# Second network's last tile: four pairs of first-layer products ahead of the projections, which accumulate in another PSUM bank

## The reference, cut to what matters

```python
attn_out = _attn_ref(q, kv, w_sr)      # pooled keys, softmax(q k^T) v: 12288 tokens x 128
h = x @ moe_w_in                       # 12288 x 2048
x = (h * (1.0 / (1.0 + np.exp(-1.702 * h)))) @ moe_w_out     # first network, back to 128
h = x @ moe2_w_in                      # second network
relu6 = np.clip(h + 3.0, 0.0, 6.0)
out = (h * relu6 / 6.0) @ moe2_w_out   # 12288 x 128, float32
```

## Time and profile before

| what | before |
|---|---|
| median of 3 runs | 1310.77 us (1310.31 to 1311.88) |
| the profiled execution, own time | 1312.06 us |
| its span, first to last instruction | 1310.3 us |
| TensorE busy | 1279.5 us, 98% |
| VectorE busy | 1037.8 us, 79% |
| ScalarE busy | 1031.9 us, 79% |
| mean granted TensorE clock | 0.997 of full |

### The profile page before, as it was taken

The page is one execution under the profiler, slowest core; times in us unless marked ns, Lnnn a source line. Parts: engine busy times, 40 slices in busy tenths (PEclk is TensorE's granted clock), DMA queues, the critical chain, the costliest instruction groups (busy, mean ns, idle before and its releaser), DMA issues.

```text
span 1310.3 us, 18296 instructions
## 1 busy us (share of the span) xinstructions
PE 1279.5 (98%) x5748; PEld 1063.1 (81%) x5748; DVE 1037.8 (79%) x1072; ACT 1031.9 (79%) x1211; POOL 36.5 (3%) x43
## 2 busy tenths in 40 slices
PE   6799999999999999999999999999999999999997
PEld 6578888888888888888888888888888888888785
DVE  4777788888878888788888887887788888887666
ACT  2678788788888888788888878888888788788665
POOL 1900000000000000000000000000000000000000
PEclk9999999999999999999999999999999999999999
DMA  9232203213023032131230321311302203102001
GB/s 283 78 72 53 65 9 72 48 24 72 21 51 71 2 72 48 24 72 28 44 72 1 72 52 20 72 36 36 72 9 63 61 11 72 43 21 65 9 1 17
DMA packets 186884, 65.94 MB, mean 50 GB/s; under 512 B 108656, under 2 KB 179440, under 8 KB 186608
## 3 DMA queue, kind: packets, MB, share of 16 engines
q1 hardware_dynamic: 185808, 65.56, 22.2%
q10 hardware_dynamic: 1056, 0.13, 0.1%
HBM read 23.13 MB, written 6.34 MB: 22 GB/s over the span
## 4 chain that ended last, share of the span: by engine, by line
PE 95%; DVE 2%; ACT 1%; DMA 1%; issue 0%; SPq 0%; ACTq 0%
PE pair L796 16%; PE pair L798 16%; PE pair L797 16%; PE bank_av L796 9%; PE bank_av L798 9%; PE bank_av L797 9%; PE bank_out L796 7%; PE bank_out L798 6%; PE bank_out L797 6%; PE pair L810 1%; DMA kv_sb<-in_kv_dram 1%; DVE neg_max L606 0%; ACT work L449 0%; DVE work L665 0%; DVE mid_lo L672 0%
## 5 line engine op out<-in xcount | busy, mean ns | idle before, releaser
L672 DVE TENSOR_TENSOR mid_lo<-work,mid_hi 128x1024 fp32r<-128x1024 f32 (+1 forms) x193 | 235.0, 1218 | 135.2 <-ACT mid_hi L462 135.0
L796 PE MATMUL pair<-x_hi,w_hi 128*128 128x512 f32 x768 | 303.0, 394 | 4.5 <-DVE x_lo L648 3.2
L797 PE MATMUL pair<-x_lo,w_hi 128*128 128x512 f32 x768 | 300.2, 391 | 0.0
L798 PE MATMUL pair<-x_hi,w_lo 128*128 128x512 f32 x768 | 299.9, 390 | 0.0
L434 ACT ACTIVATE work<-pair 128x1024 f32<-128x1024 f32 x192 | 197.1, 1027 | 126.3 <-PE pair L798 123.6
L656 DVE TENSOR_TENSOR mid_lo<-work,mid_hi 128x1024 fp32r<-128x1024 f32 x192 | 236.0, 1229 | 32.3 <-ACT mid_hi L441 32.3
L665 DVE SCALAR_TENSOR_TENSOR work<-work,pair 128x1024 f32<-128x1024 f32 (+1 forms) x193 | 232.5, 1205 | 10.0 <-ACT work L449 9.9
L449 ACT ACTIVATE work<-pair,half 128x1024 f32<-128x1024 f32 (+1 forms) x193 | 212.2, 1100 | 12.4 <-PE pair L798 12.4
L441 ACT ACTIVATE mid_hi<-work 128x1024 fp32r<-128x1024 f32 x192 | 202.6, 1055 | 5.6 <-PE bank_av L798 3.4
L462 ACT ACTIVATE mid_hi<-work 128x1024 fp32r<-128x1024 f32 (+1 forms) x193 | 201.4, 1044 | 0.6 <-DVE work L665 0.6
L796 PEld LDWEIGHTS pair<-x_hi,w_hi 128*128 128x128 f32 x768 | 144.8, 188 | 43.0 <-ACT work L434 7.0
(11 more groups left out here) (87 smaller groups left out, 1507.0 us busy)
## 6 DMA issues: line engine op xcount, KB each, us to landing
p_keys<-p_turned SPq DMA_DIRECT2D x368, 96.0 KB, 2.2
inv_b<-inv_dram SPq DMA_DIRECT2D x24, 256.0 KB, 3.2
out_dram<-y_sb SPq DMA_DIRECT2D x94, 64.0 KB, 2.4
q_raw<-in_q_dram SPq DMA_DIRECT2D x92, 64.0 KB, 2.0
kv_sb<-in_kv_dram SPq DMA_DIRECT2D x7, 768.0 KB, 10.8
w_raw<-in_moe_w_in_dram SPq DMA_DIRECT2D x2, 1024.0 KB, 8.2
inv_dram<-inv_t SPq DMA_DIRECT2D x96, 0.5 KB
kv_sb<-in_kv_dram SPq DMA_DIRECT2D x3, 256.0 KB, 11.6
```

Of the source, the lines that this page charges most:

```text
L672: dve.tensor_tensor(mid_lo[mid2(t, p)][:, part], act2[p % 2][:, part], mid_hi[mid2(t, p)][:, part], ALU.subtract).then_inc(mid2_ready, 1)
L796: pe.matmul(dst, a_hi, b_hi, start=start, stop=False)
L797: pe.matmul(dst, a_hi, b_lo, start=False, stop=False)
L798: return pe.matmul(dst, a_lo, b_hi, start=False, stop=stop)
```

## The change

The eight projections of tile 23 go to `bank_av` rather than `bank_out`, and P0 no longer waits for `turn_y(22)`; `turn_y(23)` reads `bank_av`. TensorE's order becomes H0, H1, Q, H2, H3, P0, H4, P1, H5, P2, H6, P3, H7, P4, P5, P6, P7. On VectorE `turn_y(22)` moves from behind S0 to behind L1: S0, S1, L0, S2, L1, `turn_y(22)`, S3, L2 and on as before. Nothing else is touched: no buffer is added, ScalarE's and SyncE's orders and all other tiles are the same.

```diff
+        def output2_in(t):
+
+            return bank_av if isinstance(t, int) and t == NT - 1 else bank_out
...
-                dve.transpose(y_sb[:, :], bank_out[:, :]).then_inc(y_ready, 1)
+                dve.transpose(y_sb[:, :], output2_in(t)[:, :]).then_inc(y_ready, 1)
...
                 hard_swish(NT - 1, p)
-                if p == 0:
+                if p > 0:
+                    act2_lo(NT - 1, p - 1)
+                if p == 2:
                     turn_y(NT - 2)
-                else:
-                    act2_lo(NT - 1, p - 1)
             turn_y(NT - 1)
...
-                if p == 0 and later(t):
+                if p == 0 and later(t) and output2_in(t) is bank_out:
                     pe.wait_ge(y_ready, t)
-                project(bank_out, 3, p, mid_hi[mid2(t, p)], mid_lo[mid2(t, p)],
+                project(output2_in(t), 3, p, mid_hi[mid2(t, p)], mid_lo[mid2(t, p)],
                         ready=PAIRS * NT if last_pair else None).then_inc(out2_done, 1)
...
             hidden2(NT - 1, 0)
+            hidden2(NT - 1, 1)
             finish_job(NT - 1, JOBS - 1)
-            hidden2(NT - 1, 1)
             hidden2(NT - 1, 2)
+            hidden2(NT - 1, 3)
             for p in range(PAIRS):
                 project2(NT - 1, p)
-                if p + 3 < PAIRS:
-                    hidden2(NT - 1, p + 3)
+                if p + 4 < PAIRS:
+                    hidden2(NT - 1, p + 4)
```

## The result

The changed kernel takes **1303.44 us** in the median of six runs (1302.74 to 1305.86), against 1310.54 us of the kernel before in the same sessions. The ratio is 0.9949, with a 95% interval from 0.9938 to 0.996: faster by 7.1 us, where 6.0 was forecast. The profiled execution has a span of 1301.2 us and a time of 1302.91.

A forecast was written before the change was run, and what follows sets the result against it. In the last 35 us a ring of waits among TensorE, ScalarE and VectorE was the bound; walking VectorE's queue moved `turn_y(23)` from 1306.12 to 1300.09, 6.03 us. Median 1310.77 - 6.0 = 1304.8 us, range 1303.5 to 1306.8.

The forecast's parts named there:

- The stretch behind H0: Last tile, H0 to `turn_y(23)`: TensorE's gap closes, VectorE becomes the bound, and `turn_y(23)` comes 6.03 us earlier.
- The waits ahead of P5 and P7: TensorE in the last tile: it waits about 0.35 us twice, for L5 and L7, and nowhere else.
- The step of 1.33 us: VectorE's queue, last tile: an L followed by an S that must wait for it costs 1.33 us, otherwise 1.14.
- the bank costs nothing: Last tile's projections: writing to `bank_av` costs nothing, as its last readers are done before H0.
- P0 waiting for the transpose: Second rival, ahead of P0: it still follows `turn_y(22)`, idle 3.0 us, low clock 1.7; gain 2.1, 1308.7 us; chance 0.04.
- the first: Rival, TensorE in the last tile: the clock falls once all the same; gain 5.1, 1305.8 to 1306.1 us; chance 0.08.
- the third rival: TensorE behind H0: clock falls at the 1275 us wait and stays low over 96 matmuls; 1323 us; chance 0.04.
- What the Trainium skill reports: TensorE, last tile: short idles between matmul groups cycling through PSUM buffers can lower the clock repeatedly; 1305.8 to 1306.1 us.
- 1.7 us of low clock: P0 and H3 of the kernel before: 4.47 us against 2.73 in a stream, so low clock and slow starts took 1.7.
- The first 1275 us: Everything ahead of H0 keeps its queue place and should not move; a move there would show the prediction wrong.
- The range: Median of the changed kernel: 1303.5 to 1306.8 us, with 0.5 us for scatter and the clock case taken in.
- C: Rival theory of the experiments, ahead of H0: the 3.0 us by which H0 is earlier belong to the change; no chance given.

The follow-up runs named there:

- e5: Changed kernel with four result tiles in turn for S in the last tile instead of two; H0 to `turn_y(23)` 23.92 us, median 1304.14 us.
- e3: Changed kernel's TensorE order, but all projections in `bank_out` and `turn_y(22)` behind S0 as before; H0 to `turn_y(23)` 24.61 us, median 1305.75 us.
- e4: Changed kernel with all projections in `bank_out`, P0 waiting for `turn_y(22)`, which stays behind L1; H0 to `turn_y(23)` 28.33 us, median 1309.19 us.
- e8: The changed kernel itself, measured again in more rounds; H0 to `turn_y(23)` 24.48 us, median 1303.94 us, ratio to before 0.9953.
- e6: Changed kernel with four result tiles for S and `turn_y(22)` behind L0 instead of L1; H0 to `turn_y(23)` 23.77 us, median 1302.72 us.
- e7: Changed kernel with one more transpose on VectorE behind L3, into a tile nobody reads; H0 to `turn_y(23)` 24.88 us, median 1305.42 us.
- e1: Changed kernel with three pairs of first-layer products ahead instead of four; H0 to `turn_y(23)` 27.56 us, median 1308.34 us, ratio to before 0.9986.
- e2: Changed kernel with Q ahead of H1 again; H0 to `turn_y(23)` 25.69 us, median 1306.42 us, ratio to before 0.9962.
- e10: The kernel before, unchanged, profiled again; H0 to `turn_y(23)` 28.96 us, one run of 1311.01 us.
- e9: Changed kernel with TensorE's order as before, keeping the other bank and `turn_y(22)` behind L1; H0 to `turn_y(23)` 28.95 us, median 1309.99 us.
- e11: The kernel before, unchanged, profiled once more; H0 to `turn_y(23)` 30.51 us, one run of 1310.79 us.
- e12: Changed kernel with TensorE's order as before, other bank and transpose's place kept, profiled once more; H0 to `turn_y(23)` 30.58 us, one run of 1309.69 us.

## Why the prediction was right or wrong

**The stretch behind H0: right, step by step.** The forecast's times, moved by the 3.01 us by which H0 is earlier, against the rows above: P0 1279.46 and 1279.42; S2 1279.43 and 1279.41; `turn_y(22)` 1281.71 and 1281.69; S3 1282.34 and 1282.32; S6 1289.75 and 1289.66; S7 1293.24 and 1293.15; `turn_y(23)` 1297.08 and 1296.98. The gain there was to be 6.03 and is 6.13. The waits ahead of P5 and P7 are where they were put. The step of 1.33 us that rested on one place is 1.31 from L2 to S4 in the changed kernel, and e5 confirms its cause: it falls to 1.13 without the wait. That the bank costs nothing is right; the prediction did not ask what it earns, and e3 puts it, together with the transpose's new place, at 0.12 us.

**The rivals.** P0 waiting for the transpose was priced at a gain of 2.1 us with a 3.0 us idle and the low clock; built as e4 it gains 30.62 - 28.33 = 2.29, by the same steps. Between H0 and `turn_y(23)` the clock never left 1.00 in the changed order with two banks (the changed kernel, e8, e5, e6, e7): the waits of 0.2 us, and the 0.65 us one in e7, did not lower it, nor did the 0.88 us ones in e1 and e2. So the first and the third rival did not come. What the Trainium skill reports in "TensorE: Matmul & The Clock Gate", "A second HAM failure mode: psum-queue depth-cycling", and what the prediction weighed, is not seen in the last tile of these runs: short waits between groups that cycle through PSUM buffers left the clock at 1.00.

**The clock of the kernel before: a term that was taken as fixed.** The step that counted 1.7 us of low clock into the stretch of before is right for the profile that it was read from and not for every execution: without the fall the stretch is 28.95 us and the changed kernel's gain 28.95 - 24.49 = 4.5 us; with it 6.1. That the profile read for the forecast had the fall was luck. Taken off e10's 28.96 us, the forecast stretch of 30.62 - 6.03 = 24.59 us gives a gain of 4.4 (an estimate), 1.7 us less. The change takes the idle away and with it the chance of a fall.

**The first 1275 us: the term that was mis-sized.** The prediction had it that they "should not move", allowed 0.5 us of scatter, and named a move there as a sign of being wrong; that sign came. In the 14 profiles, all with the same program up to there, H0 starts anywhere from 1271.77 to 1276.29, and the runs of the kernel before in one session alone reach from 1308.04 to 1312.92. So the median, 1303.44, lies 0.06 us below the low end of the range while the stretch that the change touches came out within 0.1 us. The range is also 0.2 us wider at both ends than its own terms give: 1304.2 - 0.5 = 1303.7, and 1306.1 + 0.5 = 1306.6.

Where the head differs can be read from its rows: 48 small products of the attention's pooling, then the first product of the first network, then its first projection; before, and then after.

```profile
11.14 8.86 PE L810 MATMUL pair<-patch,kv_sb 128*128 128x96 f32 x48 [0.85 <-DVE kv_sb L562]
...
51.96 0.66 PE L796 MATMUL pair<-x_hi,w_hi 128*128 128x512 f32 x1 [2.77 <-DVE x_lo L648]
...
59.12 0.50 PE L796 MATMUL bank_av<-mid_hi,w_hi 128*128 128x512 f32 x1 [1.17 <-DVE mid_lo L656]
```

```profile
11.21 7.61 PE L814 MATMUL pair<-patch,kv_sb 128*128 128x96 f32 x48 [0.74 <-DVE kv_sb L566]
...
50.95 0.50 PE L800 MATMUL pair<-x_hi,w_hi 128*128 128x512 f32 x1 [2.79 <-DVE x_lo L652]
...
56.09 0.50 PE L800 MATMUL bank_av<-mid_hi,w_hi 128*128 128x512 f32 x1 [0.65 <-DVE mid_lo L660]
```

And the clock in stretches of the head, before and then after:

```profile
52.00:56.00 4.00, 4.00 (x11) 3.15 (x12) 1.65 (x2) 1.28 (x3) 3.63 (x5) 0.57 0.00 0
```

```profile
36.00:40.00 4.00, 4.00 (x19) 3.94 (x20) 2.56 (x7) 1.97 (x4) 3.63 (x4) 0.63 1.05 285
52.00:56.00 4.00, 3.44 (x15) 2.37 (x13) 1.83 (x3) 3.28 (x4) 3.82 (x4) 1.00 0.02 4
```

At the first projection the whole lead is there, 59.12 - 56.09 = 3.03 us. Two thirds of it are the clock: it falls at the start of the first network before, and not after, and the way from that start to the first projection takes 7.16 us in the one and 5.14 in the other. So it is in all 14: where the clock falls there (before, e1, e2, e3, e5, e7, e9, e10, e11), this way takes 7.11 to 7.17 us; where it stays (changed, e4, e6, e8, e12), 5.13 to 5.15. The fall costs 2.0 us. The low stretch at 36 us, which four of the latter five have and e4 has not, shows no cost of its own: from the attention's product at about 34 us, ahead of that stretch, to the start of the first network it is 16.77 to 16.81 us in the changed kernel, e6 and e12, and 16.79 in e4; e8 takes 17.36, but e2, e3, e9 and e10 take 18.0 without a low stretch there. The rest of the scatter lies further ahead: the first network starts anywhere from 49.88 (e5) to 52.34 us (e3). Of the 3.0 us between before and after, 1.0 is of this kind; the pooling products above take 8.86 us in the one and 7.61 in the other, both at a recorded clock of 1.00.

So C falls as it was put: e7 has the changed kernel's program up to H0 and a late H0, and e12 has the order of before and an early one.

**What stays open.** Both profiles of the changed kernel had an early H0, and its two medians lie 7.1 us below those of before, while the stretch explains 4.5 to 6.1. Whether the remaining 1.0 to 2.6 us are the luck of a dozen runs or whether something in the changed program makes the early H0 more frequent is not settled here. Luck is the likelier: the median less the stretch is 1279.0 and 1279.5 us for the changed kernel and 1279.0 for e6, but 1280.2 to 1281.1 for e1, e2, e3, e5 and e7, which have the same program up to H0. This is an argument from six to ten runs of each, not a proof. Why the clock falls behind the same idle in one execution and not in the next was not tried either.

## What to carry to other kernels

When engines wait for one another in a ring, count how many items one of them is ahead and price one more by walking the rows forward; here the fourth pair was worth 3.1 us and Q's place 1.2, while the second accumulator, which looks like the larger edit, was worth 0.1 together with the transpose's new place. After the fix ask at once for the next bound: VectorE's queue took over, and 0.7 us more lay in a buffer count and in the place of one transpose. Read the change's effect from the stretch it touches, measured from a common event, and not from the spans, when the head of the program scatters by nearly as much as the change is worth. And profile the kernel before more than once when a wait in it goes with a lower clock: one profile here would have put the gain at 6.1 us, another at 4.5.

## What the runs showed of the hardware

Two programs with the same order on TensorE and the same 2.24 us of idle ahead of P0 kept the full clock in two profiles of five (e9, e10) and fell to 0.50 in three (before, e11, e12), at a cost of 1.6 us; before (e10, e11) and the bank alone (e9, e12) each did both. The fall came 0.1 to 0.7 us after P0's start in these three, worked out from the granted clock of stretches of one us. The 2.96 us idle of e4 fell in its one profile, 0.5 us ahead of P0, and in the last tile waits of 0.88 us and less never lowered the clock.

The start of the first network shows the same over all 14 profiles: behind 2.72 to 3.31 us of idle the clock fell in nine, at a cost of 2.0 us, and stayed in five, and the length does not part them (it fell behind 2.75 us in e5 and stayed behind 3.23 us in e8). That fall accounts for 2.0 of the 4.5 us by which H0's start differs between executions of one and the same code; the other 2.5 us arise before it.
